# A fused attention and two-layer kernel: scores and states of both halves share a PSUM bank each, and the state products follow the scores at once

## The chip, the cores and the metric

One core of one Trainium2 chip runs the kernel. The metric is the device time of one execution in microseconds. A profile is one further execution under the hardware profiler; its span is the time between its first and last instruction. The kernel before took 830.83 us (median of three runs, 828.88 to 831.17).

## The reference

The input goes through three layers. The first is a linear attention with a decaying state, for 4 sequences (batch), 8 heads, 768 tokens and 48 dimensions a head:

```python
for t in range(S):
    kt, vt, rt = (k[:, :, t], v[:, :, t], r[:, :, t])
    cur = np.einsum('bhd,bhe->bhde', u[None] * kt, vt)
    y[:, :, t] = np.einsum('bhd,bhde->bhe', rt, state + cur)
    state = w[None, :, :, None] * state + np.einsum('bhd,bhe->bhde', kt, vt)
```

The second is a feed-forward layer over the 3072 tokens, 384 to 2048 and back: `h = x @ w_in`, `g = max(h, 0) + alpha * min(h, 0)`, `g @ w_out`. The third gives each token to one of 8 experts by its gate values (at most 384 tokens each, the largest values first) and applies `max(x @ w1[e], 0) @ w2[e]`.

## The kernel before, in words

The 768 tokens of a sequence are cut into 6 chunks of 128. A chunk of the attention is computed for the four batches `b` one after the other, for all 8 heads at once. Within a chunk the recurrence is replaced by products over two halves `j` of 64 tokens. For each chunk `c` and batch `b` TensorE does these small products:

- `scores(c, b)` (L1160): for 8 heads and 2 halves, decayed keys times decayed queries, 48 rows deep, 64x64 each. Half 0 uses rows 64 to 111 and columns 0 to 63 of the array, half 1 rows 0 to 47 and columns 64 to 127 (`heads_in`, `halves`). 16 products, which the trace shows as 32 records.
- `new_state(c, b)` (L1179): padded keys times values, 64 rows deep, 48x48 each, again 16 products and 32 records; half 0 lies on rows 0 to 63 and columns 64 to 111, half 1 on rows 64 to 127 and columns 0 to 47.
- `attend(c, b)` (L1193): the values' products. Masked scores and decayed queries, stacked to 128 rows, times values and state; the two halves go to different partitions of one bank.
- `turn(c, b)` (L1214): three 128x128 transposes of the result, the input of the feed-forward layer.

VectorE masks the scores (`mask`, L753, both halves one after the other), adds what `attend` gave (`attended`), carries the state from half to half (`update(c, b, 0)` at L777 and `update(c, b, 1)` at L784) and scales keys and queries (`scale_k` L730, `scale_r` L743). GpSimd makes the padded keys (L404), decays the state and makes low parts of operands.

The feed-forward layer of chunk `i` (512 tokens) is what TensorE's time goes to: 16 hidden tiles `f`. `hidden(i, f)` (L1229) and `back(i, f)` (L1242, the down projection) are 9 matmuls of 128x512 each (three products of high and low parts, L1156 to L1158). VectorE makes the activation of a tile (q at L897, g at L900), ScalarE its high part gh (L586), GpSimd its low part gl (L455).

The order on TensorE is written out by hand in `chunk` (L1268): while the feed-forward layer of chunk `i` runs, the attention of chunk `i + 1` is put between its tiles. Batch `b` has the tiles 4b to 4b + 3, and behind hidden tile `f` comes one group:

```python
(scores, new_state, attend, turn)[f % 4](i + 1, f // 4)
```

followed by `output_tile` (chunks from 1 on, at f % 4 == 2) and, from tile 2 on, by `back(i, f - 2)`. Chunk 0's feed-forward layer has the first five tiles apart (`early`): scores of chunk 1, batch 0, behind tile 1, its state products behind tile 2, `attend` at tile 3, `turn` at tile 4, then the scores of batch 1. The attention of chunk 0 itself runs alone at the start, with groups of idle matmuls between (`busy`). The experts follow behind chunk 5 and are not touched.

PSUM has eight banks of 128 x 512 fp32. From chunk 1 on half 0 of the scores and, later, of the state uses bank 5, half 1 of both bank 6 (`score_bank`, `state_bank`). Since the state products reuse the scores' banks they wait until the scores are masked (`masked`), and the next batch's scores wait until VectorE has read the state (`s_updated`).

Of the kernel before, what the change touches and what calls it, by code (L numbers as in the profile page):

```python
# [30 lines left out]
def build(nc, rT, kT, rN, kN, v, wT, uR, w_in, w_out, alpha, w_gate, w1, w2, out):  # L31
# [15 lines left out]
    with ExitStack() as ctx:  # L47
# [3 lines left out]
        def sem(name):  # L51
            return ctx.enter_context(nc.semaphore(name))

        banks = [ctx.enter_context(nc.psum_tensor(f"bank{i}", [P, 512], F32)) for i in range(8)]
# [120 lines left out]
        scores_done, masked, y_done, x_ready = sem("scores_done"), sem("masked"), sem("y_done"), sem("x_ready")  # L175
        s_decayed, s_decayed2, state_done, s_updated = sem("s_decayed"), sem("s_decayed2"), sem("state_done"), sem("s_updated")
# [45 lines left out]
        def first(c):  # L222
            return isinstance(c, int) and c == 0


        def halves(j):

            return slice(j * HALF, j * HALF + HALF)

        def heads_in(j):  # L230

            return slice((1 - j) * HALF, (1 - j) * HALF + D)

        def y_bank(c, b):
            return banks[6 if b == B - 1 else 0] if first(c) else banks[7]

        def score_bank(c, b, j):
            return banks[1 + j] if first(c) and b == 1 else banks[5 + j]

        def state_bank(c, b, j):  # L240
            return banks[(1 if b % 2 else 3) + j] if first(c) else banks[5 + j]

        def weights(c, b):
            if not first(c) or b % 2 == 0:
                return both
            return (g[:], q[:])[b // 2].rearrange("p d (h t) -> p d h t", h=H)
# [5 lines left out]
        def turn_bank(c, b):  # L252
            return banks[5 if first(c) and b == 2 else 7][:, 0:DM].rearrange("p (k t) -> p k t", k=KD)
# [7 lines left out]
        def wait(eng, semaphore, value):  # L261

            if not isinstance(value, int) or value > 0:
                eng.wait_ge(semaphore, value)
# [431 lines left out]
        def _(dve):  # L696
# [55 lines left out]

            def mask(c, b):  # L753
                for j in range(2):
                    dve.wait_ge(scores_done, 8 * c + 2 * b + j + 1)
                    rows = halves(j)
                    nc.vector.tensor_tensor(weights(c, b)[rows, j], score_bank(c, b, j)[rows].rearrange("p (h t) -> p h t", h=H),
                                            before[rows, rows].unsqueeze(1).to_broadcast([HALF, H, HT]), ALU.mult).then_inc(masked, 1)
# [392 lines left out]
        def _(pe):  # L1151
            pe.wait_ge(consts_set, NCONST)

            def product3(o, a_h, a_l, b_h, b_l, first, last):

                nc.tensor.matmul(o, a_h, b_h, start=first, stop=False)  # L1156
                nc.tensor.matmul(o, a_h, b_l, start=False, stop=False)  # L1157
                return nc.tensor.matmul(o, a_l, b_h, start=False, stop=last)  # L1158

            def scores(c, b):  # L1160
                pe.wait_ge(rk_scaled, 12 * c + 3 * b + 3)
                if first(c):
                    if b >= 2:
                        pe.wait_ge(masked, 2 if b == 2 else 6)
                elif isinstance(c, int) and c == 1 and b == 0:
                    pe.wait_ge(masked, 8)
                    pe.wait_ge(x_ready, 4)
                else:
                    pe.wait_ge(s_updated, 8 * c + 2 * b)
                wait(pe, x2n_ready, B * (c - 2) + b + OUT_PRE)  # L1170
                wait(pe, logits_ready, B * (c - 2) + b + OUT_PRE)
                for h in range(H):
                    for j in range(2):
                        mm = nc.tensor.matmul(score_bank(c, b, j)[halves(j), h * HT:(h + 1) * HT], kt[heads_in(j), b % 2, h], weights(c, b)[heads_in(j), j, h],  # L1174
                                              start=(h == 0), stop=(h == H - 1), skip_group_check=True)
                        if h == H - 1:
                            mm.then_inc(scores_done, 1)

            def new_state(c, b):  # L1179
                pe.wait_ge(v_loaded[b], 48 * c + 48)  # L1180
                pe.wait_ge(kpad_ready, B * c + b + 1)
                if first(c) and b >= 2:
                    pe.wait_ge(s_updated, 2 * b - 2)
                else:
                    pe.wait_ge(masked, 8 * c + 2 * b + 2)
                for h in range(H):
                    cols = slice(h * D, (h + 1) * D)
                    for j in range(2):
                        mm = nc.tensor.matmul(state_bank(c, b, j)[heads_in(j), cols], kpad[halves(j), b % 2, cols], vs[halves(j), b, j, cols],  # L1189
                                              start=(h == 0), stop=(h == H - 1), skip_group_check=True)  # L1190
                mm.then_inc(state_done, 1)

            def attend(c, b):  # L1193
                pe.wait_ge(masked, 8 * c + 2 * b + 2)
                if first(c):
                    pe.wait_ge(pads_set, 3)
                    pe.wait_ge(first_state, b + 1)
                else:
                    pe.wait_ge(s_updated, 8 * c + 2 * b + 1)
                if not first(c):  # L1200
                    pe.wait_ge(xl_ready, B * c + b)
                elif b < B - 1:
                    wait(pe, x_ready, b)
                def product(h, j):
                    cols = slice(h * D, (h + 1) * D)
                    return nc.tensor.matmul(y_bank(c, b)[halves(j), cols], weights(c, b)[:, j, h], vs[:, b, j, cols],  # L1206
                                            start=(h == 0), stop=(h == H - 1), skip_group_check=True)

                for h in range(H):
                    for j in range(2):  # L1210
                        mm = product(h, j)
                mm.then_inc(y_done, 1)

            def turn(c, b):  # L1214
                if first(c):
                    pe.wait_ge(x_ready, b + 1)
                    pe.wait_ge(rk_scaled, 9)
                    if b == 2:
                        pe.wait_ge(masked, 8)
                    else:  # L1220
                        wait(pe, xl_ready, (b + 1) // 2)
                else:
                    pe.wait_ge(x_ready, B * c + b + 1)
                for k in range(KD):
                    mm = nc.tensor.transpose(turn_bank(c, b)[:, k], x[:, b % 2, k * P:(k + 1) * P], ident)  # L1225
                mm.then_inc(xt_done, 1)
# [15 lines left out]
            def back(c, f):  # L1242
                if f == 0:
                    if first(c):
                        pe.wait_ge(s_updated, 8)
                    wait(pe, x2t_act, 2 * c)
                    wait(pe, x2t_dve, c)
                if isinstance(c, int) and c == 0:
                    pe.wait_ge(stage_lo, first_use["out", f])
                pe.wait_ge(gl_ready, NF * c + f + 1)  # L1250
                for k in range(KD):
                    cols = slice(k * P, (k + 1) * P)
                    mm = product3(banks[k][:, 0:TB], wout_h[:, f, cols], wout_l[:, f, cols], gh[:, f % 2], gl[:, f % 2], f == 0, f == NF - 1)
                mm.then_inc(out_done, 1)
# [13 lines left out]
            def chunk(i, attention=True, output=True):  # L1268
                for f in range(NF):
                    hidden(i, f)  # L1270
                    early = isinstance(i, int) and i == 0 and f < 5
                    if attention and not early:
                        (scores, new_state, attend, turn)[f % 4](i + 1, f // 4)
                    if early and f == 1:
                        scores(1, 0)
                    if early and f == 2:
                        new_state(1, 0)
                    if early and f == 4:
                        turn(1, 0)
                    if output and f % 4 == 2:  # L1280
                        output_tile(i - 1, f // 4)
                    if f >= 2:
                        back(i, f - 2)
                    if early and f == 3:
                        attend(1, 0)
                    if early and f == 4:
                        scores(1, 1)
                back(i, NF - 2)
                back(i, NF - 1)

# [42 lines left out]
            c = NCH - 1  # L1333
# [194 lines left out]
```

## Time and profile before

| | |
|---|---|
| runs | 831.17, 830.83, 828.88 us |
| profiled execution | 829.7 us |
| its span | 827.9 us |
| mean granted TensorE clock | 0.974 of 2.4 GHz |
| TensorE busy | 784.0 us (95%) |
| VectorE busy | 511.9 us (62%) |
| GpSimd busy | 478.4 us (58%) |
| ScalarE busy | 209.5 us (25%) |

The profiled execution's own time exceeds its span by 1.8 us, which lie outside the first and last instruction. Attention of chunk 0 ends at about 40 us, the five chunks of feed-forward with attention beside them last to about 440 us, chunk 5's feed-forward without attention follows, and the experts run from about 550 us on. A matmul's duration in a row includes its way through the array, so successive matmuls overlap; what one costs is read from the distance between starts.

### The profile page before, as it was taken

How to read it: one execution, taken by the hardware profiler on the slowest of the kernel's cores; microseconds unless marked ns; L12 is line 12 of the kernel's file. 1: busy time of each engine (PE TensorE's matmuls, PEld its weight loads, DVE VectorE, ACT ScalarE, POOL GpSimd, SP SyncE). 2: the span in 40 equal slices, each digit the busy share in tenths (PEclk: the TensorE clock that was granted, in tenths of full speed). 3: DMA queues.
4: the chain of work that ended last, by engine and by line, in shares of the span. 5: the costliest groups of instructions: out<-in, count | busy, mean ns of one | idle time of the engine just before them, and what ended most of it. 6: DMA issues, size and time to landing. Idle time of an engine off the chain costs nothing.

```text
span 827.9 us, 15950 instructions
## 1 busy us (share of the span) xinstructions
PE 784.0 (95%) x6317; PEld 654.8 (79%) x6325; DVE 511.9 (62%) x1038; ACT 209.5 (25%) x432; POOL 478.4 (58%) x471
## 2 busy tenths in 40 slices
PE   5789999999999999999999999938999999999996
PEld 4578778888788878887888888715889989989996
DVE  7867666666666666666665334477777777776221
ACT  1323312111111121111111211104244344353451
POOL 6888975555555555554553343207476775775881
PEclk8999999999999999999999999958999999999999
DMA  7855421222222222222000000014514505518401
GB/s 213 217 166 142 140 74 53 65 65 68 68 68 69 68 62 64 67 68 68 29 11 11 15 15 10 10 41 180 182 49 163 209 20 193 173 38 280 141 20 38
DMA packets 46649, 75.17 MB, mean 91 GB/s; under 512 B 6256, under 2 KB 31984, under 8 KB 46576
## 3 DMA queue, kind: packets, MB, share of 16 engines
q1 hardware_dynamic: 38176, 56.66, 21.8%
q10 hardware_dynamic: 5328, 8.06, 3.5%
q0 software_dynamic: 3072, 9.44, 3.2%
q8 instruction: 50, 0.82, 0.4%
q14 instruction: 23, 0.19, 0.1%
HBM read 64.71 MB, written 9.44 MB: 90 GB/s over the span
## 4 chain that ended last, share of the span: by engine, by line
PE 82%; DVE 9%; issue 3%; POOL 3%; DMA 2%; ACT 2%; SPq 0%; POOLq 0%; DVEq 0%; ACTq 0%
PE bank L1156 23%; PE bank L1158 21%; PE bank L1157 21%; PE bank L1174 3%; PE bank L1206 3%; PE bank L1264 2%; PE bank L1189 2%; POOL gl L455 2%; PE bank L1394 2%; DVE grid L1052 2%; PE bank L1337 2%; DVE grid L1050 1%; PE bank L1225 1%; DMA rt<-rT 1%; PE bank L1404 1%
## 5 line engine op out<-in xcount | busy, mean ns | idle before, releaser
L455 POOL TENSOR_TENSOR gl<-g,gh 128x512 fp32r<-128x512 f32 x96 | 126.0, 1313 | 211.9 <-ACT gh L586 211.9
L897 DVE TENSOR_SCALAR q<-bank,alpha_sb 128x512 f32<-128x512 f32 x96 | 72.0, 751 | 145.3 <-PE bank L1158 145.3
L586 ACT CAST gh<-g 128x512 fp32r<-128x512 f32 x96 | 59.6, 621 | 367.7 <-PE bank L1158 335.0
L1156 PE MATMUL bank<-gh,wout_h 128*128 128x512 f32 x288 | 120.1, 417 | 0.7 <-POOL gl L455 0.2
L1156 PE MATMUL bank<-xTh,win_h 128*128 128x512 f32 x288 | 113.9, 396 | 0.3 <-DVE xTl L790 0.3
L1158 PE MATMUL bank<-gh,wout_l 128*128 128x512 f32 x288 | 112.8, 392 | 0.0
L1157 PE MATMUL bank<-gl,wout_h 128*128 128x512 f32 x288 | 112.7, 391 | 0.0
L1157 PE MATMUL bank<-xTl,win_h 128*128 128x512 f32 x288 | 112.6, 391 | 0.0
L1158 PE MATMUL bank<-xTh,win_l 128*128 128x512 f32 x288 | 112.6, 391 | 0.0
L524 POOL TENSOR_TENSOR w1l<-raw,w1h 128x384 fp32r<-128x384 f32 x64 | 65.5, 1023 | 28.9 <-ACT w2h L643 28.7
L1156 PE MATMUL bank<-xeh,w1h 128*128 128x384 f32 x192 | 69.7, 363 | 0.5 <-DVE xel L984 0.5
L1156 PE MATMUL bank<-w2h,gh 128*128 128x384 f32 x192 | 68.5, 357 | 0.1
L900 DVE SCALAR_TENSOR_TENSOR g<-bank,q 128x512 f32<-128x512 f32 x96 | 66.4, 692 | 3.3
L525 POOL TENSOR_TENSOR w2l<-raw,w2h 128x384 fp32r<-128x384 f32 x64 | 65.8, 1028 | 0.0
L1156 PEld LDWEIGHTS bank<-gh,wout_h 128*128 128x128 f32 x288 | 54.1, 188 | 13.9 <-POOL gl L455 2.6
L514 POOL DMA_INDIRECT xg<-x2rows,idx x24 | 23.3, 969 | 71.7 <-DVE idx L1015 66.6
L1157 PE MATMUL bank<-xel,w1h 128*128 128x384 f32 x192 | 64.7, 337 | 0.0
L1158 PE MATMUL bank<-xeh,w1l 128*128 128x384 f32 x192 | 64.6, 336 | 0.0
L1158 PE MATMUL bank<-w2h,gl 128*128 128x384 f32 x192 | 64.6, 336 | 0.0
L1157 PE MATMUL bank<-w2l,gh 128*128 128x384 f32 x192 | 64.5, 336 | 0.0
L1156 PEld LDWEIGHTS bank<-xTh,win_h 128*128 128x128 f32 x288 | 54.4, 189 | 12.5 <-DVE xTl L790 0.8
L1158 PEld LDWEIGHTS bank<-gh,wout_l 128*128 128x128 f32 x288 | 54.1, 188 | 11.8
(176 smaller groups left out, 1498.9 us busy)
## 6 DMA issues: line engine op xcount, KB each, us to landing
raw<-w SPq DMA_DIRECT2D x32, 768.0 KB
kt<-kT SPq DMA_DIRECT2D x48, 96.0 KB, 2.7
rt<-rT SPq DMA_DIRECT2D x48, 96.0 KB, 2.8
vs<-v SPq DMA_DIRECT2D x48, 96.0 KB, 2.9
vn<-v SPq DMA_DIRECT2D x24, 192.0 KB, 3.1
x2rows<-x2n SPq DMA_DIRECT2D x24, 192.0 KB, 1.9
kn<-kN SPq DMA_DIRECT2D x20, 192.0 KB, 2.4
rn<-rN SPq DMA_DIRECT2D x20, 192.0 KB, 2.6
```

The costliest lines, as they stand in the source:

```text
L455: nc.gpsimd.tensor_tensor(gl[:, f % 2], g[:, f % 2], gh[:, f % 2].bitcast(F32), ALU.subtract).then_inc(gl_ready, 1)
L514: nc.gpsimd.indirect_dma_start(xg[:, a, :], None, x2rows, bass.IndirectOffsetOnAxis(ap=idx[:, p, a:a + 1], axis=0)).then_inc(gathered[a], 16)
L524: nc.gpsimd.tensor_tensor(w1l[:, f], raw1[:, p % 2, :, f * P:(f + 1) * P], w1h[:, f].bitcast(F32), ALU.subtract).then_inc(wlo1_ready, 1)
L525: nc.gpsimd.tensor_tensor(w2l[:, f], raw2[:, p % 2, f, :], w2h[:, f].bitcast(F32), ALU.subtract).then_inc(wlo_ready, 1)
L586: nc.scalar.copy(gh[:, f % 2], g[:, f % 2]).then_inc(gh_ready, 1)
L897: nc.vector.tensor_scalar(q[:, f % 2], h, 0.0, alpha_sb[:, f:f + 1], ALU.min, ALU.mult).then_inc(q_ready, 1)
L900: nc.vector.scalar_tensor_tensor(out=g[:, f % 2], in0=h, scalar=0.0, in1=q[:, f % 2], op0=ALU.max, op1=ALU.add).then_inc(g_ready, 1)
L1156: nc.tensor.matmul(o, a_h, b_h, start=first, stop=False)
L1157: nc.tensor.matmul(o, a_h, b_l, start=False, stop=False)
L1158: return nc.tensor.matmul(o, a_l, b_h, start=False, stop=last)
L1174: mm = nc.tensor.matmul(score_bank(c, b, j)[halves(j), h * HT:(h + 1) * HT], kt[heads_in(j), b % 2, h], weights(c, b)[heads_in(j), j, h], ...
L1206: return nc.tensor.matmul(y_bank(c, b)[halves(j), cols], weights(c, b)[:, j, h], vs[:, b, j, cols], start=(h == 0), stop=(h == H - 1), ski ...
```

## The change

From chunk 1 on both halves' scores go to bank 5 and both halves' state products to bank 6. The state products therefore no longer need the mask to be done; they wait for the state update of the batch before, and the scores for its mask. In the order of `chunk`, the state products stand directly behind the scores, at f % 4 == 0, and there is no group at f % 4 == 1. In chunk 0's early tiles the state products of chunk 1, batch 0 move from tile 2 to tile 1, and those of batch 1 follow their scores at tile 4. The mask waits for the scores of both halves before its first half. Chunk 0's own attention is as before.

```diff
         def score_bank(c, b, j):
-            return banks[1 + j] if first(c) and b == 1 else banks[5 + j]
+            return banks[(1 if b == 1 else 5) + j] if first(c) else banks[5]
 
         def state_bank(c, b, j):
-            return banks[(1 if b % 2 else 3) + j] if first(c) else banks[5 + j]
+            return banks[(1 if b % 2 else 3) + j] if first(c) else banks[6]
...
             def mask(c, b):
                 for j in range(2):
-                    dve.wait_ge(scores_done, 8 * c + 2 * b + j + 1)
+                    dve.wait_ge(scores_done, 8 * c + 2 * b + (j + 1 if first(c) else 2))
...
                     if b >= 2:
                         pe.wait_ge(masked, 2 if b == 2 else 6)
-                elif isinstance(c, int) and c == 1 and b == 0:
-                    pe.wait_ge(masked, 8)
-                    pe.wait_ge(x_ready, 4)
                 else:
-                    pe.wait_ge(s_updated, 8 * c + 2 * b)
+                    pe.wait_ge(masked, 8 * c + 2 * b)
+                    if c == 1 and b == 0:
+                        pe.wait_ge(x_ready, 4)
...
                 if first(c) and b >= 2:
                     pe.wait_ge(s_updated, 2 * b - 2)
-                else:
-                    pe.wait_ge(masked, 8 * c + 2 * b + 2)
+                elif first(c):
+                    pe.wait_ge(masked, 2 * b + 2)
+                elif c > 1 or b > 0:
+                    pe.wait_ge(s_updated, 8 * c + 2 * b)
...
                     if attention and not early:
-                        (scores, new_state, attend, turn)[f % 4](i + 1, f // 4)
+                        if f % 4 == 0:
+                            scores(i + 1, f // 4)
+                            new_state(i + 1, f // 4)
+                        if f % 4 == 2:
+                            attend(i + 1, f // 4)
+                        if f % 4 == 3:
+                            turn(i + 1, f // 4)
                     if early and f == 1:
                         scores(1, 0)
-                    if early and f == 2:
                         new_state(1, 0)
...
                     if early and f == 4:
                         scores(1, 1)
+                        new_state(1, 1)
```

TensorE, a batch in the middle of a chunk, before: the last two matmuls of hidden tile f % 4 == 0 (L1157, L1158), the scores (L1174), and the start of the down projection's tile (L1156 and on, reading gh and gl).

```order
L1157 MATMUL bank<-xTl,win_h 128x512
L1158 MATMUL bank<-xTh,win_l 128x512
L1174 MATMUL bank<-both,kt 64x64 [waits x2n_ready,logits_ready,s_updated,rk_scaled]
L1174 MATMUL bank<-both,kt 64x64 x15
L1156 MATMUL bank<-gh,wout_h 128x512 [waits gl_ready]
L1157 MATMUL bank<-gl,wout_h 128x512
```

Eighteen big matmuls further, behind the next hidden tile, before:

```order
L1157 MATMUL bank<-xTl,win_h 128x512
L1158 MATMUL bank<-xTh,win_l 128x512
L1189 MATMUL bank<-vs,kpad 48x48 [waits masked,kpad_ready,v_loaded2]
L1189 MATMUL bank<-vs,kpad 48x48 x15
L1156 MATMUL bank<-gh,wout_h 128x512 [waits gl_ready]
L1157 MATMUL bank<-gl,wout_h 128x512
```

The first of the two places with the change (scores L1173, state products L1190):

```order
L1157 MATMUL bank<-xTl,win_h 128x512
L1158 MATMUL bank<-xTh,win_l 128x512
L1173 MATMUL bank<-both,kt 64x64 [waits x2n_ready,logits_ready,masked,rk_scaled]
L1173 MATMUL bank<-both,kt 64x64 x15
L1190 MATMUL bank<-vs,kpad 48x48 [waits s_updated,kpad_ready,v_loaded2]
L1190 MATMUL bank<-vs,kpad 48x48 x15
L1156 MATMUL bank<-gh,wout_h 128x512 [waits gl_ready]
L1157 MATMUL bank<-gl,wout_h 128x512
```

The state products have moved ahead of 18 big matmuls. Behind the second hidden tile the down projection's tile now follows directly. On VectorE, ScalarE, GpSimd and SyncE the order of the instructions is the same in both kernels.

## Rows read from the trace of the kernel before

**Rows 1.** The page, part 1: busy time, share of the span, instructions

```profile
PE 784.0 (95%) x6317; PEld 654.8 (79%) x6325; DVE 511.9 (62%) x1038; ACT 209.5 (25%) x432; POOL 478.4 (58%) x471
```

**Rows 2.** Stretches: busy us (instructions) of each engine, TensorE's clock, DMA share, GB/s

```profile
140.00:230.00 90.00, 89.90 (x734) 72.46 (x732) 56.55 (x82) 15.18 (x29) 47.29 (x43) 1.00 0.22 68
```

**Rows 3.** Timeline of TensorE, 250 to 258 us: start, duration, engine, line

```profile
250.74 0.39 PE L1158 MATMUL bank<-xTh,win_l 128*128 128x512 f32 x1
251.06 1.15 PE L1174 MATMUL bank<-both,kt 48*64 48x64 f32 x32
...
252.47 0.39 PE L1157 MATMUL bank<-gl,wout_h 128*128 128x512 f32 x1
...
254.31 0.39 PE L1156 MATMUL bank<-xTh,win_h 128*128 128x512 f32 x1
...
256.12 0.39 PE L1158 MATMUL bank<-xTh,win_l 128*128 128x512 f32 x1
256.44 0.92 PE L1189 MATMUL bank<-vs,kpad 64*48 64x48 f32 x32
...
257.63 0.39 PE L1157 MATMUL bank<-gl,wout_h 128*128 128x512 f32 x1
```

**Rows 4.** Durations of single matmuls (ns min/median/max), 240 to 262 us; timeline around the transposes

```profile
L1206 PE MATMUL bank<-vs,both x46: 222/222/257, 240.6 to 262.0; 128*64 128x48 f32 x46
L1174 PE MATMUL bank<-both,kt x32: 218/218/267, 251.1 to 252.0; 48*64 48x64 f32 x32
L1189 PE MATMUL bank<-vs,kpad x32: 205/205/240, 256.4 to 257.2; 64*48 64x48 f32 x32
...
246.29 0.39 PE L1158 MATMUL bank<-xTh,win_l 128*128 128x512 f32 x1
...
247.09 0.39 PE L1157 MATMUL bank<-gl,wout_h 128*128 128x512 f32 x1
```

**Rows 5.** Chunk 0: timeline of TensorE, durations of its second scores, one stretch

```profile
15.25 1.98 PE L1174 MATMUL bank<-g,kt 48*64 48x64 f32 x32 [0.51 <-DVE g L743]
17.02 1.49 PE L1189 MATMUL bank<-vs,kpad 64*48 64x48 f32 x32
...
29.33 1.14 PE L1206 MATMUL bank<-vs,both 128*64 128x48 f32 x32 [0.37 <-DVE both L757]
30.40 0.92 PE L1189 MATMUL bank<-vs,kpad 64*48 64x48 f32 x32
...
L1174 PE MATMUL bank<-g,kt x32: 311/311/367, 15.3 to 16.9; 48*64 48x64 f32 x32
...
15.00:17.00 2.00, 1.75 (x32) 0.50 0.87 271
```

**Rows 6.** Timeline at the start of chunk 1: TensorE, then VectorE

```profile
131.49 0.39 PE L1158 MATMUL bank<-xTh,win_l 128*128 128x512 f32 x1
...
134.93 1.14 PE L1206 MATMUL bank<-vs,both 128*64 128x48 f32 x32
...
131.92 0.75 DVE L897 TENSOR_SCALAR q<-bank,alpha_sb 128x512 f32<-128x512 f32 x1 [0.56 <-PE bank L1158]
...
133.43 0.56 DVE L777 TENSOR_TENSOR vs<-bank,decayed 48x384 f32<-48x384 f32 x1
```

**Rows 7.** Timeline ahead of the scores at 251 us: GpSimd, then VectorE

```profile
243.46 1.46 POOL L404 TENSOR_TENSOR kpad<-kn,knpow 128x384 f32<-128x384 f32 x1
...
248.23 0.55 DVE L784 TENSOR_TENSOR vs<-bank,decayed 48x384 f32<-48x384 f32 x1
```

**Rows 8.** Chunk 1's first scores: timeline of TensorE, and one stretch

```profile
47.15 1.47 PE L1174 MATMUL bank<-both,kt 48*64 48x64 f32 x32 [2.13 <-DVE both L743]
...
49.15 0.63 PE L1157 MATMUL bank<-xTl,win_h 128*128 128x512 f32 x1
49.58 0.63 PE L1158 MATMUL bank<-xTh,win_l 128*128 128x512 f32 x1
...
48.60:50.90 2.30, 2.30 (x8) 0.50 0.30 94
```

## The prediction

> **What bounds the kernel now.** I read the page first. TensorE is busy for 784 of 827.9 us [rows 1]. The table by stretches shows that this average hides no hole in the main loop: from 140 to 230 us (chunks 1 and 2) TensorE is busy 89.90 of 90 us at the full clock, VectorE 57, GpSimd 47, ScalarE 15 [rows 2]. There only TensorE's own stream counts, and a wait that disappears on another engine is worth nothing. TensorE's one long wait in the loop is 2.1 us before the scores of chunk 1, batch 0 [rows 8].
>
> "Busy" hides something, though, which the timeline of single matmuls shows [rows 3]. The starts of the big 128x512 matmuls are 0.226 us apart (eight steps from 254.31 to 256.12). A group of small products between two of them costs more than its own matmuls:
> - Scores: the last big matmul before starts at 250.74, the second one behind at 252.47: 1.73 us, less two normal steps (0.45) = 1.28 us for the slot. Its 32 records last 0.218 us each and start (1.15 - 0.218)/31 = 0.030 us apart, so they fill 32 x 0.030 = 0.96. The other **0.32 us** are the way in and out.
> - State products: 256.12 to 257.63 is 1.51, less 0.45 = 1.06 us. Steps of (0.92 - 0.205)/31 = 0.023, 32 of them 0.74; again **0.32 us** of way in and out.
> - The three transposes (full 128x128 form) in the same kind of place: 246.29 to 247.09 is 0.80, less 0.45 = 0.35 us for all three, ways included [rows 4]. If 0.32 of that were way, 0.01 us would be left for each 128-column product. So the 0.32 us belongs to the change between the full array and the small tiles.
>
> **The change, part by part.** No matmul, no byte and no VectorE, ScalarE, GpSimd or SyncE instruction is added, removed or reordered. TensorE's order changes, two banks are used differently, and some waits are others.
>
> *1. The state products follow the scores directly, 20 times* (chunks 1 to 5, four batches). The two slots cost 1.28 + 1.06 = 2.34 us now. Together they take: way in 0.32 (250.74 to 251.06), starts of the scores 0.93, the step from the last score to the first state product, starts of the state products 0.715, and from the last of these (256.44 + 0.715 = 257.155) to the second big one 0.475, less two steps, 0.45. Without the step in the middle that is 1.99. This step is not in the loop of the trace; the near rows are in chunk 0 [rows 5]. There state products stand right behind scores at half clock: the last score starts at 15.25 + 1.98 - 0.31 = 16.92, the first state product at 17.02, 0.10 us where a step within was 0.054. And behind the values' products (128-row tiles, so the tile form changes too) at full clock: 29.33 + 1.14 - 0.22 = 30.25 to 30.40, 0.15 us. The lowest is a plain step, 0.03. I take 0.08, nearest to the row with the same two kinds: 2.07 us together, **a gain of 0.27 us**, times 20 = 5.4 us (4.0 with 0.15, 6.4 with 0.03).
>
> *2. The slot one hidden tile later becomes empty.* Where a product of the down projection lies between, VectorE has time. But at the start of chunks 1 to 4 none stands between hidden tiles 1 and 2, and the values' products behind tile 2 wait for the first state update, which VectorE makes behind the activation of tile 1. Now [rows 6] tile 1's last matmul starts at 131.49, VectorE begins on it at 131.92 and ends the update at 133.99, and the values' products start at 134.93: 0.94 us of slack. The moved slot was 1.06 us of the time between. Computed forward, with both groups behind tile 0: tile 1 ends 2.07 - 1.28 = 0.79 us later than now, the update at 134.78, and tile 2 would let the values' products start at 134.93 - 0.27 = 134.66. With 0.05 to 0.1 us for the semaphore that is a **new stall of about 0.2 us**, 4 times: 0.8 us lost (0.5 to 1.2).
>
> *3. Waits.* The scores no longer wait for the state update of the batch before; the state products now do. That costs nothing: the update ended at 248.78, 2.3 us before the scores start [rows 3, 7]. The padded keys end at 244.92 on GpSimd, 6 us before [rows 7]. The state products no longer wait for the mask. The mask's first half now waits for the scores of both halves, one step of 0.03 us, while VectorE is still in the activation. Behind a waiting state product only big matmuls are queued, and neither of its operands is late. SyncE's queue keeps its order and its signals.
>
> *4. The first tiles of chunk 1.* The 2.1 us wait before the scores at 47.15 stays; behind it TensorE runs at half clock until 50.9, big matmuls in steps of 0.43 us [rows 8]. State products move into that stretch and big matmuls out of it. At half clock the state group took 1.49 us instead of 0.92 [rows 3, 5], about 0.5 us more, and in that time some three big matmuls leave, which gain 0.2 us each: nothing on balance.
>
> *5. Both halves in one bank.* The halves of the scores use different rows and different columns of the array, in turn. Now they write two banks, then one, on different partitions. Below: nothing, as for the values' products, whose halves do share a bank, though each uses all rows: (1.14 - 0.222)/31 = 0.0296 us a step against 0.0301 for the scores [rows 3, 4, 6]. Above: that a half must wait for the other. A 128-column fp32 transpose takes 0.35/3 = 0.117 us [rows 4], so 64 columns alone would take 0.058 and 48 columns 0.044; steps of 0.030 and 0.023 show that the halves overlap. I take nothing, since the nearest row with one bank shows nothing.
>
> The Trainium skill speaks against this edit: "TensorEngine Tiling (Array Packing)", section Restrictions and Gotchas, says that different row tiles cannot access the same PSUM bank simultaneously, and that software has to see to it. No row of this trace has two row tiles in one bank. By that rule the overlap would be lost, and the sum would be the one of the first rival. "PSUM — Partial Sum Buffer", section on bank collisions, narrows the collisions that were measured to one bank and one 32-partition quadrant, which these halves do not share; by that the sum stands.
>
> **Sum:** -5.4 + 0.8 = -4.6 us. The profiled execution took 829.7 us, so 825.1. It lay 1.1 below the median of the runs (830.8) and 0.4 below the mean of all four (830.1); I take the mean and forecast **825.5 us**, with 823 to 827.5 from the bounds and the spread of the runs. 0.3%, about what a measurement of this kernel can tell from no change, is 2.5 us.
>
> **Rivals.**
> - *One bank makes the halves take turns (slower).* Place: the 20 x 64 = 1280 matmul records of the double slots. Full price: 32 x (0.058 - 0.030) + 32 x (0.044 - 0.023) = 0.90 + 0.67 = 1.57 us, times 20 = 31 us: 825.5 + 31 = **857 us**. It decides from 4.6/1280 = 3.6 ns a record on, and from 5.5 ns the kernel is slower by over 0.3%. For it: the overlap is real in the rows. Against it: the values' products lose nothing in one bank. Chance 0.11.
> - *The way in and out is not saved (no change).* If the array has to empty between scores and state products as well, the step between them costs what the ways cost, 0.32 + 0.03, and only the new stall is left: 830.1 + 0.8 = **831 us**; with half of it 828. The 0.10 us step in chunk 0 speaks against it, though it stands at half clock. Chance 0.12.
> - *The clock stays low longer in chunk 1's first tiles.* Small products fill the low stretch where big ones did. A second one of 3.8 us (47.1 to 50.9) costs 3.8 x (1 - 0.226/0.43) = 1.8 us: **827.3 us**. In chunk 0 scores and state products ran at half clock from 15 to 17 us and beyond [rows 5]. Chance 0.07.
>
> **How the numbers follow.** The forecast has 0.70. Faster by over 0.3% (below 827.6): that and 0.03 of the clock's case, 0.73. Within 0.3%: the other 0.04 of it and 0.10 of the second rival, 0.14. Slower: the first rival and 0.02 of the second, 0.13. The range 822.8 to 829.5 holds the forecast, the clock's case and part of the second rival, some 0.8.
>
> **What would show it.** In the changed profile the first state product should start about 0.08 us behind the last score, and the double slot measure 2.07 us. Steps of 0.030 and 0.023 inside the groups refute the first rival; 0.05 and 0.04 would prove it. TensorE should gain a wait of about 0.2 us at the values' products near the start of chunks 1 to 4, put down to VectorE's state update. A middle step near 0.3 us, a stall longer than 0.5 us, or a new wait for padded keys would make the forecast wrong.

## The result, and the profile after

| | before | changed |
|---|---|---|
| median | 829.89 us (828.88 to 831.17, 4 runs) | 822.54 us (821.79 to 823.35, 4 runs) |
| ratio | | 0.9907 (95%: 0.9889 to 0.9926) |
| profiled execution | 829.7 us | 821.81 us |
| its span | 827.9 us | 819.8 us |
| TensorE's mean clock in the span | 0.974 | 0.982 |

The kernel became 7.35 us faster. The prediction said 825.5, with 822.8 to 829.5 (its sum alone: 823 to 827.5): right in sign, with 60% of the size, and 0.26 us outside the wider range. The chip ran the changed kernel once more in a later comparison: 823.44 us against 829.47, ratio 0.9923 (0.9908 to 0.9938). The two comparisons give 7.4 us (6.1 to 9.2 by the ratio's interval) and 6.0 us (5.1 to 7.6). Part of the first figure was the clock of single executions, as the loops below show.

The first two rows are the page of the changed kernel, part 1 (busy us, share, instructions) and its clock over 40 slices.

```profile
PE 775.4 (95%) x6317; PEld 654.4 (80%) x6325; DVE 515.2 (63%) x1038; ACT 209.7 (26%) x432; POOL 478.4 (58%) x471
...
PEclk9999999999999999999999999958999999999999
```

TensorE has the same 6317 instructions as in [rows 1] and is busy for 8.6 us less. The timeline of TensorE in the changed kernel shows the double slot, where [rows 3] had one group (start, duration, engine, line):

```profile
245.96 0.39 PE L1158 MATMUL bank<-xTh,win_l 128*128 128x512 f32 x1
246.27 1.15 PE L1173 MATMUL bank<-both,kt 48*64 48x64 f32 x32
247.25 0.89 PE L1190 MATMUL bank<-vs,kpad 64*48 64x48 f32 x32
248.07 0.50 PE L1156 MATMUL bank<-gh,wout_h 128*128 128x512 f32 x1
248.41 0.40 PE L1157 MATMUL bank<-gl,wout_h 128*128 128x512 f32 x1
```

Read as before: 245.96 to 248.41 is 2.45 us, less two steps = **2.00 us** for both groups (2.34 in two slots before, 2.07 forecast). The last score starts at 246.27 + 1.15 - 0.218 = 247.20, the first state product at 247.25: the step between the groups is 0.05 us. The steps inside are (1.15 - 0.218)/31 = 0.030 and (0.89 - 0.205)/31 = 0.022, no longer than in [rows 3] and [rows 4].

These 0.030 us are only a mean. The single records start in pairs, one record of each half (both records of the last pair of scores signal `scores_done`, which each half's last product does once). The counts of records begun in growing stretches show it, first for the scores (L1173), then for the state products (L1190): the stretch, its length, TensorE's busy us (records), then weight loads, clock, DMA share and GB/s.

```profile
246.20:247.15 0.95, 0.88 (x30) 0.88 (x32) 1.00 0.63 205
246.20:247.19 0.99, 0.92 (x30) 0.92 (x32) 1.00 0.64 211
246.20:247.21 1.01, 0.94 (x32) 0.94 (x32) 1.00 0.65 210
...
247.22:247.27 0.05, 0.01 (x2) 0.05 (x4) 1.00 0.90 338
247.22:247.29 0.07, 0.04 (x2) 0.07 (x4) 1.00 0.88 329
247.22:247.31 0.09, 0.06 (x4) 0.09 (x5) 1.00 1.01 376
```

To the nanosecond the pairs start at 247.138 and 247.145, at 247.197 and 247.203 (the last scores), and at 247.255 and 247.262 (the first state products). Within a pair the halves are 0.007 us apart; from one pair to the next it is 0.052 us, and the step from the last score to the first state product is these same 0.052 us. So going from one group on tiles to the other costs nothing beyond a plain step. The first rival falls too: the two halves start 0.007 us apart into one bank, as they did into two, and lose nothing.

The Trainium skill's "TensorEngine Tiling (Array Packing)", section Restrictions and Gotchas, which says that different row tiles cannot access the same PSUM bank simultaneously, does not hold here in that width: the halves, on different rows, columns and partitions, keep their steps of 0.030 us and start 0.007 us apart. No run here puts two row tiles on the same partitions of a bank at once.

At the start of chunk 1 [rows 6] the stall is there. TensorE, then VectorE, in the changed kernel:

```profile
131.09 0.39 PE L1158 MATMUL bank<-xTh,win_l 128*128 128x512 f32 x1
131.65 1.14 PE L1207 MATMUL bank<-vs,both 128*64 128x48 f32 x32 [0.17 <-issue]
...
130.98 0.56 DVE L777 TENSOR_TENSOR vs<-bank,decayed 48x384 f32<-48x384 f32 x1
```

The update ends at 131.54, and the values' products start at 131.65, 0.56 us behind the last hidden matmul's start instead of the 0.32 of a way in: 0.24 us lost, four times. The profile puts the gap down to "issue"; that it is this wait is shown by an experiment.

The clock is the third difference. Where TensorE ran at half clock in [rows 8], this execution did not (busy us and count of TensorE, clock, DMA share, GB/s):

```profile
45.00:47.10 2.10, 0.09 (x2) 1.00 0.69 222
47.10:48.60 1.50, 1.50 (x60) 1.00 0.58 191
48.60:50.90 2.30, 2.30 (x23) 1.00 0.32 95
```

The wait ahead is no shorter: TensorE stands idle for 2.3 us before the scores, where it was 2.13 in [rows 8]. The execution of the later comparison had the half clock:

```profile
47.10:48.60 1.50, 1.42 (x38) 0.76 0.63 223
48.60:50.90 2.30, 2.30 (x35) 0.50 0.29 86
```

That makes a comparison of like with like possible. From the first hidden matmul to the last group of output_tile, which lies in chunk 5 (in the kernel before the chunks with attention beside them last to 464.7 us, not to about 440 as said above), in the kernel before, in the changed one's first profile, and in the later one:

```profile
40.61 0.50 PE L1156 MATMUL bank<-xTh,win_h 128*128 128x512 f32 x1 [0.30 <-DVE xTl L790]
...
521.89 0.86 PE L1264 MATMUL bank<-id_wg,x2T 128*128 128x136 f32 x6
```

```profile
40.30 0.50 PE L1156 MATMUL bank<-xTh,win_h 128*128 128x512 f32 x1 [0.30 <-DVE xTl L790]
...
514.09 0.85 PE L1265 MATMUL bank<-id_wg,x2T 128*128 128x136 f32 x6
```

```profile
40.66 0.50 PE L1156 MATMUL bank<-xTh,win_h 128*128 128x512 f32 x1 [0.30 <-DVE xTl L790]
...
515.69 0.86 PE L1265 MATMUL bank<-id_wg,x2T 128*128 128x136 f32 x6
```

The loop, from the first of these starts to the second, takes 481.28, 473.79 and 475.03 us. With the half clock in both kernels the change is worth **6.25 us**. The first profile shows 7.49, 1.24 us of which is the absent half clock.

### The profile page after: what moved, and what is told of

Same layout as the page of the kernel before. It is cut to its first block, busy times and chain, and to the rows that moved or that the text cites. A ratio compares the mean times of both kernels' runs of the same rounds, so it can differ in the third digit from the quotient of the medians.

```text
span 819.8 us, 15950 instructions
## 1 busy us (share of the span) xinstructions
PE 775.4 (95%) x6317; PEld 654.4 (80%) x6325; DVE 515.2 (63%) x1038; ACT 209.7 (26%) x432; POOL 478.4 (58%) x471
## 4 chain that ended last, share of the span: by engine, by line
PE 82%; DVE 9%; issue 3%; POOL 3%; ACT 2%; DMA 1%; POOLq 0%; SPq 0%; DVEq 0%; ACTq 0%
PE bank L1156 23%; PE bank L1158 21%; PE bank L1157 21%; PE bank L1207 3%; PE bank L1173 3%; PE bank L1190 2%; PE bank L1265 2%; POOL gl L455 2%; PE bank L1401 2%; DVE grid L1052 2%; PE bank L1344 2%; DVE grid L1050 1%; PE bank L1411 1%; PE bank L1226 1%; DMA xg<-x2rows,idx 1%
## 5 line engine op out<-in xcount | busy, mean ns | idle before, releaser
L1156 PE MATMUL bank<-gh,wout_h 128*128 128x512 f32 x288 | 118.4, 411 | 0.7 <-POOL gl L455 0.2
L1156 PE MATMUL bank<-xTh,win_h 128*128 128x512 f32 x288 | 113.0, 392 | 0.3 <-DVE xTl L790 0.3
L1157 PE MATMUL bank<-gl,wout_h 128*128 128x512 f32 x288 | 112.6, 391 | 0.0
L1158 PE MATMUL bank<-gh,wout_l 128*128 128x512 f32 x288 | 112.5, 391 | 0.0
L1157 PE MATMUL bank<-xTl,win_h 128*128 128x512 f32 x288 | 112.2, 389 | 0.0
L1158 PE MATMUL bank<-xTh,win_l 128*128 128x512 f32 x288 | 112.1, 389 | 0.0
L1156 PE MATMUL bank<-xeh,w1h 128*128 128x384 f32 x192 | 69.7, 363 | 0.5 <-DVE xel L984 0.5
L1156 PE MATMUL bank<-w2h,gh 128*128 128x384 f32 x192 | 68.5, 357 | 0.1
L1156 PEld LDWEIGHTS bank<-gh,wout_h 128*128 128x128 f32 x288 | 54.1, 188 | 13.4 <-POOL gl L455 2.6
L1157 PE MATMUL bank<-xel,w1h 128*128 128x384 f32 x192 | 64.6, 337 | 0.0
L1158 PE MATMUL bank<-xeh,w1l 128*128 128x384 f32 x192 | 64.6, 336 | 0.0
L1158 PE MATMUL bank<-w2h,gl 128*128 128x384 f32 x192 | 64.6, 336 | 0.0
L1157 PE MATMUL bank<-w2l,gh 128*128 128x384 f32 x192 | 64.5, 336 | 0.0
L1156 PEld LDWEIGHTS bank<-xTh,win_h 128*128 128x128 f32 x288 | 54.0, 188 | 12.2 <-DVE xTl L790 0.8
L1158 PEld LDWEIGHTS bank<-gh,wout_l 128*128 128x128 f32 x288 | 54.1, 188 | 11.9
```

## The experiments

Twelve runs in three sets, eleven new kernels and the changed one again; each set had its own runs of the kernel before. Besides the medians, which differ by 1 to 2 us with the clock, I compare the loop's length (as above) and the distance between two groups of output_tile inside a chunk, a batch's period. It is 178.09 - 157.04 = 21.05 us in the kernel before:

```profile
157.04 0.96 PE L1264 MATMUL bank<-id_wg,x2T 128*128 128x136 f32 x6
178.09 0.96 PE L1264 MATMUL bank<-id_wg,x2T 128*128 128x136 f32 x6
```

and 196.48 - 175.80 = 20.68 us in the changed one (its later execution; the first has 20.68 too), **0.37 us less a batch**:

```profile
175.80 0.96 PE L1265 MATMUL bank<-id_wg,x2T 128*128 128x136 f32 x6
196.48 0.96 PE L1265 MATMUL bank<-id_wg,x2T 128*128 128x136 f32 x6
```

**Banks without the order.** The order of before on the banks and waits of the change:

```diff
-                        if f % 4 == 0:
-                            scores(i + 1, f // 4)
-                            new_state(i + 1, f // 4)
...
+                        (scores, new_state, attend, turn)[f % 4](i + 1, f // 4)
...
+                    if early and f == 2:
                         new_state(1, 0)
...
```

> The changed kernel with the order of before: both halves' scores in bank 5, both halves' states in bank 6, the waits of the change, but the state products one hidden tile behind the scores. Theory (the gain is the way into and out of the small tiles, saved once per pair): no gain, 829 to 831 us, slots of 1.28 and 1.06 us as before, steps of 0.030 and 0.023. Rival (one bank instead of two, or the looser waits, give a part of the gain): 1 to 7 us less. Rival (one bank costs something that the merge hides): 1 us or more above before.

830.75 us (829.74 to 831.73, 11 runs) against 830.5 us (828.03 to 831.78, 27 runs); ratio 1.0012 (1.0001 to 1.0022). Its loop is 521.93 - 40.66 = 481.27 us, where before had 481.28. The median is 0.25 us higher and the ratio's interval just leaves out 1, but the loop shows none of it. Banks and waits alone give nothing, and one bank costs nothing that the loop could show:

```profile
250.77 0.39 PE L1158 MATMUL bank<-xTh,win_l 128*128 128x512 f32 x1
251.09 1.15 PE L1173 MATMUL bank<-both,kt 48*64 48x64 f32 x32
...
252.51 0.39 PE L1157 MATMUL bank<-gl,wout_h 128*128 128x512 f32 x1
```

**The pair split by nine big matmuls** (batches 1 to 3; batch 0 of a chunk, and batch 1 of chunk 1, as before)**.**

```diff
...
                     if f >= 2:
                         back(i, f - 2)
+                    if attention and not early and f % 4 == 0 and f > 0:
+                        new_state(i + 1, f // 4)
...
```

> The changed kernel, but for batches 1 to 3 nine big matmuls (the down projection's tile) stand between the scores and the state products; for batch 0 of a chunk, and for batch 1 of chunk 1, the state products have their old place. Banks and waits are those of the change. Theory (adjacency alone saves): all 20 pairs pay both ways again, 829 to 831 us. Rival (the state products being early helps, by state updates that come sooner): 822.5 to 826.

831.19 us (828.95 to 832.39, 11 runs), ratio 1.0005 (0.9992 to 1.0018). A batch's period is the 21.05 us of before. The state products come nine big matmuls later than in the changed kernel and nine sooner than before, and all of the gain is gone, not half of it. Adjacency it is, as the theory had it. Its loop is 523.78 - 40.91 = 482.87 us, 1.6 more than before, 1.5 of them ahead of hidden tile 5 of chunk 0: the half clock behind chunk 1's first scores lasted longer in this profile (granted clock 0.60 from 50.9 to 55 us, before 0.96); that is about the price which the prediction's third rival had named, here in a kernel with before's order at that place. The second group, with its own way in and out:

```profile
255.90 0.39 PE L1158 MATMUL bank<-gh,wout_l 128*128 128x512 f32 x1
256.22 0.92 PE L1190 MATMUL bank<-vs,kpad 64*48 64x48 f32 x32
257.07 0.50 PE L1156 MATMUL bank<-xTh,win_h 128*128 128x512 f32 x1
257.41 0.39 PE L1157 MATMUL bank<-xTl,win_h 128*128 128x512 f32 x1
```

**Idle matmuls in the wait, both kernels.**

```diff
                     if early and f == 1:
+                        busy(9, banks[0])
                         scores(1, 0)
```

> The kernel before with nine idle matmuls (bf16, 128x512, bank 0, 2.0 us at full clock) put into the 2.1 us in which TensorE waits ahead of chunk 1's first scores. Theory (1.4 us of the profiled difference was the half clock behind that wait, which some executions have and others not): no execution falls to half clock after 45 us, all runs near the lower ones of before, 828.5 to 829.2, and a spread below 0.7 us. Rival (the half clock there is no matter of the wait): two levels as before, 828.9 and 831.

828.53 us (827.81 to 829.39, 11 runs), ratio 0.9984 (0.9973 to 0.9994).

> The same nine idle matmuls in the changed kernel. Theory: all runs near the lower ones of the changed kernel, 821.5 to 822.2, and 7.0 us less than the kernel before with idle matmuls: 20 x 0.37 saved less 4 x 0.23 stalls = 6.5, and some tenths elsewhere. If part of the gain was that the change keeps the clock up behind the wait, the distance of the two with idle matmuls falls to 6.0 or less.

822.76 us (821.58 to 823.26, 5 runs), ratio 0.9916 (0.9902 to 0.993). Both profiles stay at the full clock behind the wait. Busy us of TensorE and clock, the kernel before with the idle matmuls:

```profile
45.00:47.10 2.10, 2.03 (x10) 1.00 0.81 236
47.10:48.60 1.50, 1.31 (x24) 1.00 0.87 301
48.60:50.90 2.30, 2.30 (x28) 1.00 0.35 99
```

In these profiles the half clock there goes with the wait, and it costs 481.28 - 479.91 = 1.37 us of the loop of before. The spread of the kernel before with idle matmuls is 1.6 us, not the 0.7 expected: from 14 to 20 and 34 to 40 us, ahead of the loop, the clock differs between executions too (half to full in either stretch). Between the two kernels the loops differ by 479.91 - 473.77 = 6.14 us and the medians by 5.8. The loop's 6.14 is 0.4 below the 6.5 expected, and the tenths elsewhere did not come. The median of 822.76 also lies above the 821.5 to 822.2 expected. By the expectation's own mark (6.0 or less) the medians' 5.8 speak for a share of the clock in the gain and the loops' 6.14 just against it; this pair alone does not settle it, the next run does.

**The changed kernel again.**

> The changed kernel again, for more executions. Theory (whether TensorE falls to half clock behind the wait at 45 to 47 us is chance, as likely in the changed kernel as before): median 823 to 823.5, 7.0 to 7.5 us below before. Rival (the change itself keeps the clock up there): 822.0 to 822.8, 1.5 us or more beyond the 6.3 us that the loop's slots explain, and no half clock between 45 and 55 us in the profile.

823.44 us (823.17 to 824.88, 6 runs) against 829.47 (828.93 to 832.09, 11 runs). The level is the theory's, the distance 6.0 us is smaller than its 7.0. The half clock is back in this profile. Of the eleven profiles of kernels without idle matmuls at this place, ten have it and only the first one of the changed kernel lacks it. The rival (that the change keeps the clock up) falls, and with the half clock in both kernels the loops still differ by 6.25 us; what decides it in an execution was not found.

**output_tile ahead of the values' products,** at hidden tile 2 of chunks 1 to 4:

```diff
+                        if f == 2 and output:
+                            pe.wait_ge(masked, 8 * (i + 1) + 2)
+                            output_tile(i - 1, 0)
                         if f % 4 == 2:
                             attend(i + 1, f // 4)
...
-                    if output and f % 4 == 2:
+                    if output and f % 4 == 2 and not (attention and f == 2):
                         output_tile(i - 1, f // 4)
```

> The changed kernel, but at hidden tile 2 of chunks 1 to 4 the six products of output_tile (0.9 us) stand ahead of the values' products, not behind them. Theory (these products wait 0.24 us for VectorE's first state update, four times): the wait is covered, the step from the last hidden matmul to the next group is normal, 0.9 us less than the changed kernel, 821.0 to 822.0. Rival (the 0.24 us is not a wait but the way into the small tiles): no difference, and the gap moves along.

823.24 us (822.02 to 823.87, 6 runs), ratio 0.9914 (0.9899 to 0.9929): by the medians not to be told from the changed kernel, and above the 821.0 to 822.0 expected. The loop tells it: 514.78 - 40.64 = 474.14 us, 0.89 less than the 475.03 with the same half clock, where 4 x 0.24 = 0.96 was expected. The gap behind the last hidden matmul is gone, so it was the wait for VectorE's update:

```profile
132.79 0.39 PE L1158 MATMUL bank<-xTh,win_l 128*128 128x512 f32 x1
133.01 0.86 PE L1265 MATMUL bank<-id_wg,x2T 128*128 128x136 f32 x6
133.80 1.14 PE L1207 MATMUL bank<-vs,both 128*64 128x48 f32 x32
```

**The same with the idle matmuls.**

> Out_first with the nine idle matmuls ahead of chunk 1's first scores. Theory: no half clock behind 45 us in any execution, 821.0 to 822.0 with little spread; if the changed kernel hardly ever has the half clock there, the same as out_first.

820.77 us (819.96 to 821.2, 5 runs) against 829.47: ratio **0.9884** (0.9868 to 0.9901), the fastest version tried, a little below the 821.0 to 822.0 expected, and outside the range of every run of the changed kernel (821.79 at the lowest).

**The state's halves in the other order.**

```diff
-                    for j in range(2):
+                    for j in ((1, 0) if not first(c) else (0, 1)):
                         mm = nc.tensor.matmul(state_bank(c, b, j)[heads_in(j), cols], kpad[halves(j), b % 2, cols], vs[halves(j), b, j, cols],
```

> The changed kernel, but from chunk 1 on each head's state products are issued half 1 first, so that the first state product lies on the other tile of the array than the last score. Theory (the step of 0.048 us between the groups is a plain step of 0.030 and 0.02 because both lie on the same tile): the step falls to 0.03, the time by 20 x 0.02 = 0.4 us, 822.1 to 822.6. Rival (the order of the halves is of no account): the step stays 0.048.

823.38 us (821.61 to 826.2, 6 runs), ratio 0.9914 (0.9896 to 0.9931). A miss: the first state product still starts 0.99 us behind the first score, where the changed kernel has 0.98, and the period stays 20.68. It makes no difference on which tile the next group begins. The expectation had taken the mean step of 0.030 for the plain one; there was nothing to save, since the 0.052 us from the last score to the first state product are the step between any two pairs of scores. Here too the state products start at 129.587 and 129.594, behind a last score at 129.535.

```profile
128.60 1.15 PE L1173 MATMUL bank<-both,kt 48*64 48x64 f32 x32
129.59 0.89 PE L1190 MATMUL bank<-vs,kpad 64*48 64x48 f32 x32
```

**Four probes: one idle matmul in the empty slot.** All four are the changed kernel with this at f % 4 == 1, 19 times, K and M being 128 and 128, 48 and 64, 48 and 128, 128 and 64:

```diff
+            def probe(c, b):
+                pe.wait_ge(xl_ready, B * c + b)
+                nc.tensor.matmul(banks[7][0:M, 0:HT], idle_b[0:K, 0:M], idle_b[0:K, 0:HT], start=True, stop=True, skip_group_check=True)
```

> The changed kernel with one idle bf16 matmul of 64 columns (all 128 rows, 128 wide, bank 7) put into the slot that the state products left, 19 times (chunk 1 batches 1 to 3, chunks 2 to 5). Its way into the stream waits for a semaphore long passed, like the small groups. Theory (a change of tile form costs, not a slot or a wait): 0.03 to 0.05 us a place, 0.6 to 1.0 us in all, 823.3 to 824.5. Rival (each group that waits on a semaphore, or each short matmul, breaks the stream): 0.3 us a place, 6 us in all.

> The same with the idle matmul on a tile: 48 rows, 64 wide. Theory: the ways in and out, 0.34 to 0.40 us a place, 6.5 to 7.5 us in all, 829.5 to 831. Rival (the price belongs to the 16 products in fp32, not to the form): as probe_full.

> The same with 48 rows but 128 wide, so that only the rows are tiled. If any change of form drains the array, as probe_tile, 6 to 7 us; if only narrow outputs cost, as probe_full.

> The same with 128 rows but 64 wide, the form of the values' products. These pay 0.33 us at their place in the profile, so 6 to 7 us in all; if only tiled rows cost, as probe_full.

| form of the one matmul | median (us) | a batch's period | more than the changed kernel's 20.68 |
|---|---|---|---|
| 128 rows, 128 wide | 825.6 (823.4 to 826.49, 7 runs) | 20.82 | 0.14 |
| 48 rows, 64 wide | 829.71 (828.33 to 830.57, 10 runs) | 21.05 | 0.37 |
| 48 rows, 128 wide | 829.12 (827.96 to 830.69, 10 runs) | 21.04 | 0.36 |
| 128 rows, 64 wide | 829.58 (826.84 to 831.47, 10 runs) | 21.07 | 0.39 |

The medians rise less than 19 times these prices: the idle matmul at f == 1 of chunks 1 to 4 also covers the stall of 0.24 us or a part of it (one on a tile at 133.78 us, and the values' products then start 0.32 us behind the last hidden matmul). The changed kernel itself was not run in this set, so the periods are what counts. The kernel before had 830.61 us; the ratios are 0.9949 (0.9931 to 0.9967), 0.9996 (0.9981 to 1.0012), 0.9989 (0.9974 to 1.0005) and 0.9994 (0.9975 to 1.0014). The timelines of TensorE, first the full form, then the tile:

```profile
254.78 0.39 PE L1158 MATMUL bank<-xTh,win_l 128*128 128x512 f32 x1
255.01 0.20 PE L1271 MATMUL bank<-idle_b 128*128 128x64 bf16 x1
255.04 0.48 PE L1156 MATMUL bank<-gh,wout_h 128*128 128x512 f32 x1
255.36 0.40 PE L1157 MATMUL bank<-gl,wout_h 128*128 128x512 f32 x1
```

```profile
258.09 0.39 PE L1158 MATMUL bank<-xTh,win_l 128*128 128x512 f32 x1
258.41 0.21 PE L1271 MATMUL bank<-idle_b 48*64 48x64 bf16 x1
258.55 0.50 PE L1156 MATMUL bank<-gh,wout_h 128*128 128x512 f32 x1
258.89 0.40 PE L1157 MATMUL bank<-gl,wout_h 128*128 128x512 f32 x1
```

A single tiny matmul on a tile costs the whole 0.37 us that a merged pair gives back. Into it the stream takes 0.32 us instead of 0.23, out of it 0.14 instead of 0.03. Tiled rows alone or a narrow output alone cost the same. The second step behind it (0.32 to 0.34 instead of 0.23) belongs to any short matmul, also to one of the full form: there the expectation of 0.03 to 0.05 us a place was too small, it is 0.14. So of the 0.37 us, about 0.14 is the short group and 0.23 more comes with the tile form, by the difference of the two probes. What TensorE does in that time no run shows.

## Why the prediction was right or wrong

*The mechanism* (part 1: the way in and out is saved once a pair) was right: banks alone give 0, the pair split by big matmuls gives 0, one matmul on a tile takes the gain of a pair back.

*Its size* was the step that failed. The 0.27 us a pair were 0.37. Of the missing 0.10 us, 0.03 is the step between the groups: 0.05 instead of 0.08. The prediction misread the row in chunk 0 that it took this from. The records there start in pairs too. The counts of scores begun, in the kernel before, at half clock:

```profile
15.20:16.82 1.62, 1.57 (x30) 1.57 (x32) 0.50 0.87 273
15.20:16.90 1.70, 1.65 (x30) 1.65 (x32) 0.50 0.87 275
15.20:16.92 1.72, 1.67 (x32) 1.67 (x32) 0.50 0.87 275
```

The last two pairs start at 16.803 and 16.809 and at 16.909 and 16.916: from pair to pair it is 0.100 us, and the 0.10 us ahead of the first state product at 17.02 [rows 5] are that plain step. The prediction set it against the mean of 0.054 and saw a price where there was none; at full clock half of 0.10 is the 0.05 measured. Another 0.03 is the first step inside the state group, which is short when the tile form stands already (longest state product 205 ns against 240 in [rows 4]; the starts span 0.685 and not 0.715). The rest, 0.03 to 0.04, lies behind the slot, where big matmuls take 0.23 instead of 0.226 us a step for a while; I had ended the slot at the second big matmul. Over 20 pairs this is 2 us: 7.4 instead of 5.4. My upper bound of 6.4 had varied the middle step alone. With the loop's 6.25 us in place of 4.6 the forecast would have been 823.9, inside the range.

*The stall* (part 2) was right in place, cause and size: 0.24 us against about 0.2, four times; out_first took 0.89 us of it away.

*The clock* (part 4 and the third rival) was taken as a risk on one side only. I read one profile with the half clock as if all had it. It was absent from the changed kernel's first profile, 1.24 us. Two of its four executions, this one among them, had a mean clock of 0.982 and took 821.8 us; the other two had 0.972 and 0.974 and took 823.3. Had all four been like the latter, the median would lie inside the range, so the 0.26 us outside were chance on top of the size; that the second fast execution lacked the same half clock is likely, but it has no profile. With -7.4 + 1.0 = -6.4 the loop would have been forecast well: 6.25 and 6.14 were measured with like clocks. The chance of an execution without the half clock belonged in the range, about 1.4 us below.

*The first rival* (one bank makes the halves take turns) fell by the steps of 0.030 and 0.022, *the second* (way not saved) by the step of 0.05. The row that part 5 leaned on does not carry it, though: the values' products have 48 columns and a mean step of 0.0296 us, and were set against scores of 64 columns. Against state products of 48 columns, with 0.023, the step is longer by 0.007 us a record, more than the 5.5 ns from which the prediction called the kernel slower. That one bank costs nothing is known from the changed kernel's own steps and from the run with the banks alone. The argument from the transposes was half right: they show no change of form, but a short group of the full form is not free either.

*Waits* (part 3): none appeared for padded keys, for the state update at the state products or for the mask.

## What to carry to other kernels

Where small tiled products are put into a stream of full-array matmuls, count the entries and not the products: here an entry cost about 0.37 us. A lone product on a tile cost that, and merging two groups of 16 products gave it back once. Put groups on tiles side by side even if that needs another division of the banks, and then look for the wait that the emptied place no longer covers. Before a range is set from one profile, ask which of its stretches at half clock another execution would not have.

## What had not been expected of the hardware

- Only rows tiled, or only the output narrow, costs as much as both (0.36, 0.39 and 0.37 us a place).
- One 64-column matmul of the full form between big ones costs 0.14 us, five times its 0.03 us step; the loss is in the step to the second big one (0.32 us instead of 0.23).
- Products on two tiles start in pairs, 0.007 us apart within a pair and 0.052 us from pair to pair (64 columns, full clock), and the step from one group on tiles to the next is the same 0.052 us, whichever tile the second begins on.
- Half clock behind a wait of 2.1 us came in ten of eleven profiles and cost 1.2 to 1.4 us; filled with idle matmuls, the wait had none behind it in three of three. The one profile without it had waited 2.3 us.
